# One step more of lag in a software-pipelined attention: transposes, products with v and cluster ranking

## The chip, the core and the metric

The kernel runs on one core of one Trainium2 chip. The time is device microseconds (us) for one execution. The kernel before takes 794.31 us (median of 3 runs, 794.3 to 795.95). TensorE is called PE here, VectorE DVE, ScalarE ACT, GpSimd POOL, and SP is the engine that issues most DMAs.

## The reference, cut to what matters

```python
# q, k, v: (2, 8, 768, 64); centroids: (8, 16, 64)
q_assign = argmax(q_n . c_n)            # the cluster of each query, out of 16
k_assign = argmax(k_n . c_n)
scores = where(q_assign == k_assign, q k^T / 8, -1e9)
attn = softmax(scores)
x = (attn v)  ->  (1536 tokens, 512)
h = x @ w_in;  g = P(h) / Q(h);  x = g @ w_out            # first MLP, 2048 hidden
y = (silu(x @ w_gate) * (x @ w_val)) @ w_out2             # second MLP, 1536 hidden
```

All matmuls are made exact to float32 by splitting each operand into a high and a low part, so that most products are three or four matmuls.

## The kernel before

There are 16 heads (2 batches of 8). Each head has T = 6 query tiles of 128 rows against all 768 keys, so the attention is a sequence of NT = 96 tiles. One loop over `step` (lines 583, 803, 1011 and 1210) is written out once for each engine, and each engine runs its instructions strictly in that written order; semaphores join the engines. Step s handles different stages of different tiles:

- PE, from line 1210: the scores of tile s (four matmuls, L1226 and L1229; they wait for the exponentials of tile s-2), then six transposes of the probabilities of tile s-LAG (L1239), then a third of a product with v (L1254, L1256), then in some steps the cluster work of a later head.
- DVE: the row maximum of tile s (`neg_max`, L1035), once in three steps the sum and the reciprocal of three row sums (L1046, L1049, at step s divisible by three), then the low half of the transposed tile s-LAG in two instructions (`probT_lo`, L1057), and once in three steps the sum of the two parts of a finished product with v (`x_raw`, L1066).
- ACT: the exponentials of tile s-1 (L811), the high half of the transposed tile s-LAG in two instructions (`probT_hi`, L829), and once in three steps a copy of half the product with v (`x_part`, L839).
- POOL: at steps divisible by three it scales three probability tiles by their reciprocals (L589); at steps divisible by six it splits q and k of a later head (L597 to L606); at step 3 of six it splits v (L614, L617); some steps split weights of the first MLP (L624, L626); and once in twelve steps it splits the finished x of a pair of heads (L636, L638; the "x pair").

A half head is three tiles. `pv_at(step)` gives the half head g and the third whose product with v runs in a step: it starts PV_LAG = LAG + 3 steps after the half head's first scores. The first half of the transposes of a tile waits until DVE has read the first half of the tile before it out of the same PSUM bank (line 1238, semaphore s_pT_lo), and its second half likewise. The first third of a product waits for `x_raw` of the product before it (line 1251).

The cluster ranking of a head h is a chain of stages, placed by `head_at(step, stage)`: the stage runs at step 6h + late + stage - 18. Stage 6 and the step after it are the products with the cluster centres (L1313, PE), stage 8 sums them and takes the maximum (L1072 and L1074, DVE), 9 marks the maximum (L1080, DVE), 10 transposes the marks (L1278, PE), 11 ranks them (L819 on ACT, L1292 on PE) and 12 makes the cluster rows (L1024 and L1026, DVE, at the front of the step), which SP then copies to where the scores of head h read them (L390). For heads 3 and up, before the change, the centre products run at steps 0 and 1 of six, the sum at step 2, the marks at 3, their transposes at 4, the ranking at 5 and the rows at 0.

`prob` has six buffers. The exponentials of tile i overwrite the buffer of tile i-6 and wait for its transposes (line 809). They are issued in step i+1 of ACT.

At steps 96 to 103 PE also runs the first hidden units of the first MLP in pieces of six matmuls of 512 columns (TAIL_CHUNKS, L1109 to L1111). The loop ends three steps after the last product with v. The first result of the MLP (`first_result(0)`, line 1140) waits for all `x_raw` sums, since it writes the PSUM bank of the products with v. After that PE runs two long phases of matmuls.

Of the kernel before, what the change touches and what calls it, by code (L numbers as in the profile page):

```python
# [21 lines left out]
def build_program(nc, q, k, v, centroids, w_in, w_out1, a, b, w_gate, w_val, w_out2, out):  # L22
# [9 lines left out]
    HALF = T // 2  # L32
    HC = HALF * P
    NG = NH * 2
# [110 lines left out]
    def loaded(h):  # L145

        return qk_raw_3 if h == 3 else qk_raw[h % 3]
# [106 lines left out]

    R_LAG = 3
    COPIES, CLROWS = 16 * 6, 16 * T
    LAG = 5
    PV_LAG = LAG + HALF
    V_STEP = 3
    X_STEP, LAST_X_STEP = 5, 2  # L260
    PREP_LEAD = 18
    FIRST_STEP = -PREP_LEAD
    S_SPLIT, S_CEN, S_LOGIT, S_SUM, S_TOP, S_TOPT, S_RANK, S_CLUSTER = 0, 2, 6, 8, 9, 10, 11, 12
# [4 lines left out]
    def head_at(step, stage):  # L268


        for h in range(NH):
            late = -4 * (h == 1) + (h == 2 and stage <= S_SUM)
            if T * h + late == step + PREP_LEAD - stage:
                return h
        return None

    def tile_at(step):
        return step if 0 <= step < NT else None

    def pv_at(step):  # L280

        g, third = (step - PV_LAG) // HALF, (step - PV_LAG) % HALF
        return (g, third) if 0 <= g < NG else (None, None)

    def copied(h):
        return s_copy[h % 3], COPIES * (h // 3 + 1)
# [23 lines left out]
    def x_pair(x, h):  # L310
        col = (h // H) * S
        return x[:, (h % H) // 2, col:col + S]
# [51 lines left out]
    with block:  # L364
# [114 lines left out]
        def _(pool):  # L479
# [20 lines left out]
            def did(ins, signal):  # L500
                last["count", signal] = last.get(("count", signal), 0) + 1
                last["signal"] = signal
                ins.then_inc(signal, 1)

            def finish_last():


                pool.wait_ge(last["signal"], last["count", last["signal"]])

            def mlp1(n):  # L510


                i = n % 2
                if n < N1:
                    pool.wait_ge(s_lin, n + 1)
                    did(g.tensor_tensor(den[i][:, :], den[i][:, :], mag[i][:, :], ALU.mult), s_quad)  # L516
                for u, when in w1_split_at.items():
                    if when == n:
                        pool.wait_ge(s_w1_in[u], 32)
                        did(g.tensor_scalar(w1_hi[u][:, :], w1_raw[u][:, :], 1.0, 1.0, ALU.mult, ALU.mult),  # L520
                            s_w1hi)
                        pool.wait_ge(s_w1hi, u - POOL_UNITS + 1)
                        did(g.tensor_tensor(w1_lo[u][:, :], w1_raw[u][:, :], w1_hi[u][:, :].bitcast(F32),
                                            ALU.subtract), s_w1lo)
                for b, when in enumerate(T_SUM_AT):
                    if when == n:
                        token_sums(0, b)
                for m, when in enumerate(W_SUM_AT):
                    if when == n:
                        weight_sums(m)  # L530
                for k, when in enumerate(T_LO_AT):
                    if when == n:
                        token_lo(0, k)
                for m, when in enumerate(W_LO_AT):
                    if when == n:
                        weight_lo(m)
# [46 lines left out]
            for step in STEPS:  # L583
                if (step - HALF) % HALF == 0 and 0 <= (step - HALF) // HALF < NG:
                    half = (step - HALF) // HALF
                    pool.wait_ge(s_inv, half + 1)
                    for n in range(HALF):
                        i = (half * HALF + n) % T
                        did(g.tensor_scalar(prob[i][:, :], prob[i][:, :], row_inv[:, i:i + 1], 1.0,  # L589
                                        ALU.mult, ALU.mult), s_norm)  # L590
                h = head_at(step, S_SPLIT)
                if h is not None and h >= 2:
                    i = h % 3
                    if h == 2:
                        pool.wait_ge(s_qklo, 2)
                    pool.wait_ge(s_qk_in[i], 32 * (h // 3 + 1))
                    did(g.tensor_scalar(loaded(h)[0:D, :], loaded(h)[0:D, :], QSCALE, 1.0,  # L597
                                        ALU.mult, ALU.mult), s_qscale)
                    pool.wait_ge(s_qscale, h - 1)
                    if h == 3:  # L600
                        pool.wait_ge(*copied(0))
                        pool.wait_ge(s_logit, 1)
                    did(g.tensor_scalar(qk_hi[i][:, :], loaded(h)[:, :], 1.0, 1.0, ALU.mult, ALU.mult),
                        s_qkhi)
                    pool.wait_ge(s_qkhi, h + 1)
                    did(g.tensor_tensor(qk_lo[i][:, :], loaded(h)[:, :], qk_hi[i][:, :].bitcast(F32),  # L606
                                        ALU.subtract), s_qklo)

                h = (step - V_STEP) // T
                if (step - V_STEP) % T == 0 and 0 <= h < NH:  # L610
                    pool.wait_ge(s_v_in[h % 2], 16 * (h // 2 + 1))
                    if h >= 2:
                        pool.wait_ge(s_pv, 2 * (h - 1))
                    did(g.tensor_scalar(v_split[h % 2][:, :, 0, :], v_raw[h % 2][:, :, :], 1.0, 1.0,  # L614
                                    ALU.mult, ALU.mult), s_vhi)
                    pool.wait_ge(s_vhi, h + 1)
                    did(g.tensor_tensor(v_split[h % 2][:, :, 1, :], v_raw[h % 2][:, :, :],  # L617
                                    v_split[h % 2][:, :, 0, :].bitcast(F32), ALU.subtract), s_vlo)

                for u, when in pool_split_at.items():  # L620
                    if when != step:
                        continue
                    pool.wait_ge(s_w1_in[u], 32)
                    did(g.tensor_scalar(w1_hi[u][:, :], w1_raw[u][:, :], 1.0, 1.0, ALU.mult, ALU.mult), s_w1p_hi)  # L624
                    pool.wait_ge(s_w1p_hi, u + 1)
                    did(g.tensor_tensor(w1_lo[u][:, :], w1_raw[u][:, :], w1_hi[u][:, :].bitcast(F32),  # L626
                                    ALU.subtract), s_w1p)
                g1, third = pv_at(step - X_STEP)
                if pv_at(step - LAST_X_STEP) == (NG - 1, HALF - 1):
                    g1, third = NG - 1, HALF - 1  # L630
                if third == HALF - 1 and g1 % 4 == 3:
                    pool.wait_ge(s_xsum, g1 + 1)
                    finish_last()
                    h = g1 // 2
                    xh, xl, raw = x_pair(x_hi, h), x_pair(x_lo, h), x_pair(x_raw, h)
                    did(g.tensor_scalar(xh, raw, 1.0, 1.0, ALU.mult, ALU.mult), s_xhi)  # L636
                    pool.wait_ge(s_xhi, h // 2 + 1)
                    did(g.tensor_tensor(xl, raw, xh.bitcast(F32), ALU.subtract), s_xlo)  # L638
                    finish_last()

                if step in TAIL:
                    mlp1(TAIL[step])
# [15 lines left out]
        def _(sc):  # L658
# [144 lines left out]
            for step in STEPS:  # L803

                i = tile_at(step - 1)
                if i is not None:
                    sc.wait_ge(s_max, i + 1)
                    if i >= T:
# [3 lines left out]
                                 ps[:, bank:bank + 2, 0:HC], ACT.Exp, bias=neg_max[:, i % T:i % T + 1],  # L812
                                 accum_out=row_sum[:, i % T, 0:1]).then_inc(s_exp, 1)
                h = head_at(step, S_RANK)
                if h is not None:
                    sc.wait_ge(s_topT, h + 1)
                    if h == 0:
# [3 lines left out]
                                 ACT.Copy).then_inc(s_topT_in, 1)  # L821
                i = tile_at(step - LAG)
                if i is not None:
# [50 lines left out]
        def _(ve):  # L874
# [136 lines left out]
            for step in STEPS:  # L1011
# [25 lines left out]
                if (step - HALF) % HALF == 0 and 0 <= (step - HALF) // HALF < NG:  # L1037
# [11 lines left out]
                    v_.reciprocal(row_inv[:, c:c + HALF], row_den[:, c:c + HALF]).then_inc(s_inv, 1)  # L1049
                i = tile_at(step - LAG)  # L1050
                if i is not None:
# [47 lines left out]
        def _(pe):  # L1099
# [110 lines left out]
            for step in STEPS:  # L1210
                i = tile_at(step)
                if i is not None:
# [18 lines left out]
                    last.then_inc(s_score, 1)  # L1231
                i = tile_at(step - LAG)
                if i is not None:
# [143 lines left out]
```

## Time and profile before

| | |
|---|---|
| median of the runs | 794.31 us |
| the profiled execution | 794.28 us, of it a span of 792.5 us |
| PE busy | 781.2 us (99%) |
| DVE busy | 571.9 us (72%) |
| ACT busy | 517.3 us (65%) |
| POOL busy | 522.7 us (66%) |
| attention | about 16 to 264 us of the span |
| first and second MLP | about 264 us to the end |

A timeline row has the start and the busy time in us, then engine, line, operation, output and inputs, and the count of like instructions merged. A bracket at its end says how long the engine sat idle before it and what ended that. A row of matmuls counts each up to its modelled end, so the starts are what to compare: the time from one start to the next is the time that the work takes on the engine.

### The profile page before, as it was taken

The numbers are of one execution on the slowest core, as the hardware profiler recorded it, in microseconds if no ns is written. First come the engines' busy times: TensorE is split into PE (matmuls) and PEld (weight loads), VectorE is DVE, ScalarE is ACT, GpSimd is POOL, SyncE is SP. The second block draws the span as 40 slices with busy tenths as digits, with TensorE's granted clock in tenths as the row PEclk, the third lists the DMA queues.
The fourth block names the chain that finished last, engine by engine and source line by source line (L and its number), as shares of the span: only waits on it lengthen the run. The fifth ranks groups of instructions, "written<-read, shape, count | busy, mean of one in ns | idle before, by whom it ended". The sixth has DMA issues, their size and how long they took to land.

```text
span 792.5 us, 12617 instructions
## 1 busy us (share of the span) xinstructions
PE 781.2 (99%) x4204; PEld 697.7 (88%) x4204; DVE 571.9 (72%) x1043; ACT 517.3 (65%) x957; POOL 522.7 (66%) x457
## 2 busy tenths in 40 slices
PE   8999999999999999999999999999999999999998
PEld 7799999999998888888888888899999999999997
DVE  5899999999997888778777777745445545554453
ACT  4888888888887787777767889744444444333322
POOL 4767988998575799322222288888889876655620
PEclk8999999999999999999999999999999999999999
DMA  8776555454310700000000011241111114111102
GB/s 206 180 199 162 143 140 125 116 145 121 85 60 19 221 28 0 1 1 1 1 1 0 1 55 54 66 147 50 32 54 53 37 45 134 54 28 53 28 1 80
DMA packets 57681, 57.92 MB, mean 73 GB/s; under 512 B 6608, under 2 KB 44304, under 8 KB 57616
## 3 DMA queue, kind: packets, MB, share of 16 engines
q1 hardware_dynamic: 57376, 56.52, 26.6%
q8 instruction: 34, 0.56, 0.3%
q10 hardware_dynamic: 240, 0.59, 0.3%
q14 instruction: 31, 0.25, 0.1%
HBM read 33.59 MB, written 3.15 MB: 46 GB/s over the span
## 4 chain that ended last, share of the span: by engine, by line
PE 87%; DVE 8%; issue 2%; ACT 2%; DMA 0%; DVEq 0%; ACTq 0%
PE ps L1111 18%; PE ps L1109 18%; PE ps L1110 18%; PE ps L1239 6%; PE ps L1204 4%; PE ps L1205 4%; PE ps L1203 4%; DVE neg_max L1035 3%; DVE probT_lo L1057 3%; PE ps L1254 3%; PE ps L1226 3%; PE ps L1256 3%; PE ps L1313 2%; PE ps L1229 2%; ACT prob L811 1%
## 5 line engine op out<-in xcount | busy, mean ns | idle before, releaser
L516 POOL TENSOR_TENSOR den<-den,mag 128x512 f32<-128x512 f32 x48 | 62.3, 1298 | 121.8 <-ACT den L689 121.6
L1111 PE MATMUL ps<-x_hi,w_lo 128*128 128x512 f32 (+1 forms) x384 | 139.5, 363 | 0.0
L1109 PE MATMUL ps<-x_hi,w_hi 128*128 128x512 f32 (+1 forms) x384 | 139.4, 363 | 0.0
L1110 PE MATMUL ps<-x_lo,w_hi 128*128 128x512 f32 (+1 forms) x384 | 139.3, 363 | 0.0
L575 POOL TENSOR_TENSOR w_lo<-w_raw,w_hi 128x768 fp32r<-128x768 f32 (+1 forms) x48 | 101.6, 2125 | 56.4 <-ACT w_hi L742 56.4
L589 POOL TENSOR_SCALAR prob<-prob,row_inv 128x768 f32<-128x768 f32 x96 | 85.6, 907 | 39.2 <-DVE row_inv L1049 38.7
L829 ACT ACTIVATE probT_hi<-ps 128x384 fp32r<-128x384 f32 x192 | 84.2, 489 | 25.9 <-PE ps L1239 24.2
L1057 DVE TENSOR_TENSOR probT_lo<-ps,probT_hi 128x384 fp32r<-128x384 f32 x192 | 96.8, 545 | 5.3 <-ACT probT_hi L829 4.0
L1035 DVE TENSOR_REDUCE neg_max<-ps 128x1 f32<-128x768 f32 x96 | 91.1, 950 | 8.8 <-PE ps L1229 8.5
L811 ACT ACTIVATE prob<-ps,neg_max 128x768 f32<-128x768 f32 x96 | 86.8, 905 | 10.8 <-DVE neg_max L1035 10.1
L1239 PE MATMUL ps<-ident,prob 128*128 128x128 f32 x576 | 81.7, 277 | 4.4 <-DVE probT_lo L1057 4.1
L1239 PEld LDWEIGHTS ps<-ident,prob 128*128 128x128 f32 x576 | 65.6, 140 | 17.0 <-issue 9.9
L1109 PEld LDWEIGHTS ps<-x_hi,w_hi 128*128 128x128 f32 x384 | 72.1, 188 | 8.2
L1110 PEld LDWEIGHTS ps<-x_lo,w_hi 128*128 128x128 f32 x384 | 72.1, 188 | 8.2
L1111 PEld LDWEIGHTS ps<-x_hi,w_lo 128*128 128x128 f32 x384 | 72.1, 188 | 7.5
L1111 PE MATMUL ps<-g_hi,w_lo 128*128 128x512 f32 x192 | 74.8, 390 | 0.0
L1110 PE MATMUL ps<-g_lo,w_hi 128*128 128x512 f32 x192 | 74.8, 390 | 0.0
L1109 PE MATMUL ps<-g_hi,w_hi 128*128 128x512 f32 x192 | 74.8, 390 | 0.0
L1254 PE MATMUL ps<-probT_hi,v_split 128*128 128x384 f32 x192 | 72.5, 378 | 0.0
L763 ACT ACTIVATE act_hi<-ps 128x384 fp32r<-128x384 f32 x48 | 23.6, 492 | 64.6 <-DVE ps L992 43.7
L1256 PE MATMUL ps<-probT_lo,v_split 128*128 128x384 f32 x192 | 64.6, 337 | 0.0
L959 DVE TENSOR_TENSOR sum<-ps,gate 128x384 f32<-128x384 f32 x24 | 13.4, 557 | 68.9 <-PE ps L1111 68.9
(145 smaller groups left out, 1987.5 us busy)
## 6 DMA issues: line engine op xcount, KB each, us to landing
k_hihi<-qk_hi SPq DMA_DIRECT2D x32, 192.0 KB, 4.0
w_raw<-in_moe_w_gate SPq DMA_DIRECT2D x48, 128.0 KB, 2.3
w_raw<-in_moe_w_val SPq DMA_DIRECT2D x48, 128.0 KB, 2.5
w_raw<-in_moe_w_in SPq DMA_DIRECT2D x16, 256.0 KB, 3.7
w_raw<-in_moe_w_out SPq DMA_DIRECT2D x16, 256.0 KB, 5.0
qk_raw<-in_q SPq DMA_DIRECT2D x16, 192.0 KB, 3.4
q_hilo<-qk_hi SPq DMA_DIRECT2D x16, 192.0 KB, 3.4
qk_low<-qk_hi SPq DMA_DIRECT2D x16, 192.0 KB, 4.5
```

Of the source, the lines that this page charges most:

```text
L575: did(g.tensor_tensor(lo[:, wave, :], raw[:, wave, :], hi[:, wave, :].bitcast(F32), ALU.subtract), s_w2lo)
L589: did(g.tensor_scalar(prob[i][:, :], prob[i][:, :], row_inv[:, i:i + 1], 1.0, ALU.mult, ALU.mult), s_norm)
L811: s.activation(prob[i % T][:, :].rearrange("p (c n) -> p c n", c=2), ps[:, bank:bank + 2, 0:HC], ACT.Exp, bias=neg_max[:, i % T:i % T + 1] ...
L829: s.activation(probT_hi[g % 2][:, n * HALF:(n + 1) * HALF, c:c + P], ps[:, PT_BANK + n, 0:HC].rearrange("p (k n) -> p k n", k=HALF), ACT.C ...
L1035: v_.tensor_reduce(neg_max[:, i % T:i % T + 1], ps[:, bank:bank + 2, 0:HC], AX.XY, ALU.max, negate=True).then_inc(s_max, 1)
L1057: v_.tensor_tensor(probT_lo[g % 2][:, keys, c:c + P], ps[:, PT_BANK + n, 0:HC].rearrange("p (k n) -> p k n", k=HALF), probT_hi[g % 2][:, k ...
L1109: mm(dst, hi, m_hi, start=start, stop=False)
L1110: mm(dst, hi, m_lo, start=False, stop=False)
L1111: return mm(dst, lo, m_hi, start=False, stop=stop)
L1239: last = transpose(ps[:, PT_BANK + n, kt % HALF * P:(kt % HALF + 1) * P], prob[i % T][:, kt * P:(kt + 1) * P], ident[:, :])
L1254: mm(ps[:, O_BANK, 0:HC], vv, probT_hi[g % 2][:, kt, :], start=(kt == 0), stop=False)
L1256: last = mm(ps[:, O_BANK, 0:HC], vv, probT_lo[g % 2][:, kt, :], start=False, stop=(kt == T - 1))
```

## The change

Four things: LAG becomes 6, so that transposes, the halves of the transposed tile and the products with v come one step later (PV_LAG follows). The x pair of POOL comes one step after the end of its product with v instead of five, which puts it at step 9 of twelve, where v is split, in place of step 0 of twelve, where q and k are split. The special case of the last pair falls away; it stays at step 105. And for heads 2 and up all stages from the centre products on come one step later; for head 2 those up to the sum were so already.

```diff
-    LAG = 5
+    LAG = 6
     PV_LAG = LAG + HALF
     V_STEP = 3
-    X_STEP, LAST_X_STEP = 5, 2
+    X_STEP = 1
...
         for h in range(NH):
-            late = -4 * (h == 1) + (h == 2 and stage <= S_SUM)
+            late = -4 * (h == 1)
+            if h >= 2:
+                late = 1 if stage >= S_LOGIT else int(h == 2)
             if T * h + late == step + PREP_LEAD - stage:
                 return h
...
                 g1, third = pv_at(step - X_STEP)
-                if pv_at(step - LAST_X_STEP) == (NG - 1, HALF - 1):
-                    g1, third = NG - 1, HALF - 1
                 if third == HALF - 1 and g1 % 4 == 3:
```

## Rows read from the trace of the kernel before

**Rows 1.** Who waited for whom, 40 to 219 us: us in total, times, longest.

```profile
PE ps L1239 <- DVE probT_lo L1057: 3.5, 12, 0.4
```

**Rows 2.** Timeline of PE, the transposes of steps 43 to 49: start us, us.

```profile
116.57 0.82 PE L1239 MATMUL ps<-ident,prob 128*128 128x128 f32 x6
119.31 0.82 PE L1239 MATMUL ps<-ident,prob 128*128 128x128 f32 x6
121.37 0.82 PE L1239 MATMUL ps<-ident,prob 128*128 128x128 f32 x6
123.92 0.92 PE L1239 MATMUL ps<-ident,prob 128*128 128x128 f32 x6 [0.34 <-DVE probT_lo L1057]
126.31 0.82 PE L1239 MATMUL ps<-ident,prob 128*128 128x128 f32 x6
128.48 0.90 PE L1239 MATMUL ps<-ident,prob 128*128 128x128 f32 x6
131.31 0.82 PE L1239 MATMUL ps<-ident,prob 128*128 128x128 f32 x6
```

**Rows 3.** Timeline of DVE, steps 40 to 47.

```profile
110.42 1.01 DVE L1057 TENSOR_TENSOR probT_lo<-ps,probT_hi 128x384 fp32r<-128x384 f32 x2
...
112.05 0.96 DVE L1035 TENSOR_REDUCE neg_max<-ps 128x1 f32<-128x768 f32 x1
...
119.51 0.96 DVE L1035 TENSOR_REDUCE neg_max<-ps 128x1 f32<-128x768 f32 x1 [0.26 <-PE ps L1229]
120.50 1.02 DVE L1057 TENSOR_TENSOR probT_lo<-ps,probT_hi 128x384 fp32r<-128x384 f32 x2
121.44 0.36 DVE L1072 TENSOR_TENSOR ps<-ps,logit_lo 128x192 f32<-128x192 f32 x1
...
122.10 0.95 DVE L1035 TENSOR_REDUCE neg_max<-ps 128x1 f32<-128x768 f32 x1
122.97 0.15 DVE L1046 TENSOR_REDUCE row_den<-row_sum 128x3 f32<-128x6 f32 x1
...
123.24 0.99 DVE L1057 TENSOR_TENSOR probT_lo<-ps,probT_hi 128x384 fp32r<-128x384 f32 x2
124.15 0.35 DVE L1080 TENSOR_TENSOR is_top<-ps,top 128x192 f32<-128x192 f32 x1
124.42 0.95 DVE L1035 TENSOR_REDUCE neg_max<-ps 128x1 f32<-128x768 f32 x1
125.28 1.01 DVE L1057 TENSOR_TENSOR probT_lo<-ps,probT_hi 128x384 fp32r<-128x384 f32 x2
...
126.67 0.94 DVE L1035 TENSOR_REDUCE neg_max<-ps 128x1 f32<-128x768 f32 x1
```

**Rows 4.** Timeline of the end of attention, PE and DVE, steps 102 to 103 and after.

```profile
261.98 0.39 PE L1109 MATMUL ps<-x_hi,w_hi 128*128 128x512 f32 x1
...
263.41 0.47 PE L1109 MATMUL ps<-g_hi,w_hi 128*128 128x512 f32 x1
...
262.70 0.56 DVE L1066 TENSOR_TENSOR x_raw<-ps,x_part 64x384 f32<-64x384 f32 x1 [1.59 <-ACT x_part L839]
```

**Rows 5.** Timeline of PE at the start, step 4.

```profile
20.69 0.62 PE L1226 MATMUL ps<-k_hihi,q_hilo 128*128 128x384 f32 x2 [0.21 <-ACT prob L811]
...
22.84 0.42 PE L1278 MATMUL ps<-ident,is_top 128*96 128x128 f32 x2 [1.17 <-DVE is_top L1080]
```

**Rows 6.** Timeline of PE, transposes of steps 86 and 92, where no cluster work is left.

```profile
221.45 0.82 PE L1239 MATMUL ps<-ident,prob 128*128 128x128 f32 x6
...
234.35 0.82 PE L1239 MATMUL ps<-ident,prob 128*128 128x128 f32 x6
```

**Rows 7.** Timelines of POOL, PE and SP: scaling behind an x pair, and cluster rows sent.

```profile
139.53 2.69 POOL L589 TENSOR_SCALAR prob<-prob,row_inv 128x768 f32<-128x768 f32 x3
...
140.91 0.82 PE L1239 MATMUL ps<-ident,prob 128*128 128x128 f32 x6
...
118.84 4.62 SPq L390 DMA_DIRECT2D qk_low<-clusterT  x6
```

## The prediction

> **What bounds the kernel now.** I read the page first: PE is busy for nearly the whole span, also in attention. Then I asked the waits of the attention for PE's rows alone. What stands there is small and of one kind: the transposes waiting for the low half of the tile before, in the same PSUM bank [rows 1]. No wait for POOL's scaled probabilities and none for a DMA. So PE is the bound engine, and each gap is DVE running just behind it. The timeline of one head then shows where. From one start of the transposes to the next, a plain step takes PE 2.06 us (119.31 to 121.37), a step with half of the centre products 2.74 (116.57 to 119.31), the step with the mark transposes 2.39 (123.92 to 126.31), the ranking step 2.17 (126.31 to 128.48). Step 3 of six, 121.37 to 123.92, takes 2.55 for work of 2.06: a wait of 0.49 us in each head. A whole head takes 14.74 us (116.57 to 131.31) [rows 2].
>
> DVE's costs, start to start [rows 3]: row maximum 0.87 (122.10 to 122.97), sum and reciprocal 0.27 (122.97 to 123.24), the two low halves 0.94 (120.50 to 121.44) or 0.91 behind the reciprocal (123.24 to 124.15), centre sum and maximum 0.66 (121.44 to 122.10), marks 0.27 (124.15 to 124.42). The two low halves with the `x_raw` that lies between them and the next maximum take 1.39 (125.28 to 126.67), but 1.63 in another head (110.42 to 112.05). Two lags join the engines: the maximum starts 0.20 after the transposes of its step (119.31, 119.51), and the next transposes start 0.68 after the low halves (123.24, 123.92) [rows 2, 3].
>
> **The change part by part.** No instruction is added or removed. What counts is where PE stands idle, at the end, at the start, in the 13 heads that run with cluster work beside them, and in the last 12 tiles, which run without.
>
> *The end.* All PE work is the same, so an idle PE is the whole cost. Before, behind the last third of the last product with v, PE still has a piece of the MLP from 261.98 on, and under it ACT and DVE make the last `x_raw` (262.70). The first MLP result starts at 263.41, 1.43 us later, at nearly no wait [rows 4]. After the change the product ends one step later, at step 104, and there is no piece at 104: it has run ahead of it. So the 1.43 us is bare, less a few hundredths that were bare before: +1.4 us. Nothing later gives it back, since PE has no gap in the MLP that follows. The last x pair stays at step 105 of POOL and waits for the same `x_raw`; the MLP chain moves with it.
>
> *The start.* PE waits 1.17 us for the marks of head 2 in step 4 [rows 5]. They are now transposed in step 5, behind the scores of that step, so this wait mostly goes. Next late is the chain of scores, maximum and exponentials, on which the scores two tiles on wait (it shows as the 0.21 in the same group), and the first transposes have left this stretch, so there is less to fill it with. Bounds 0 and -1.17; I take -0.4, nearer to none, for that second reason.
>
> *Thirteen heads.* Scores, sum and reciprocal stay at their steps; transposes, low halves, `x_raw` and all cluster stages move by one. So the new thing is the order on DVE: `x_raw` now stands right ahead of the steps with the reciprocal, and the centre sum right behind one. Working it through, with time 0 at the transposes of step 2 of six: a centre step gives transposes 3 at 2.74 and maximum 3 at 2.94; low halves 3 at 2.94 + 0.87 + 0.27 = 4.08; transposes 4 at 2.74 + 2.06 = 4.80 (DVE would allow 4.76). Maximum 4 at 4.08 + 0.91 + 0.66 = 5.65, low halves 4 at 6.52, so transposes 5 at 6.52 + 0.68 = 7.20 where PE was ready at 6.86: a wait of 0.34. Maximum 5 at 6.52 + 0.94 + 0.27 = 7.73, low halves 5 at 8.60, maximum 0 at 8.60 + 1.39 = 9.99 or + 1.63 = 10.23, low halves 0 at 11.13 or 11.37. Transposes 0 at 7.20 + 2.39 = 9.59; transposes 1 at the later of 9.59 + 2.17 = 11.76 and 11.81 or 12.05; and the next step 2 at + 2.83 (the 128.48 to 131.31 of rows 2) = 14.64 or 14.88. The mean is 14.76. The same working on the order of before gives: low halves 2 at 1.07, sum 2.01, maximum 3 at 2.67, low halves 3 at 3.81, transposes 4 at 4.49, then 6.88, 9.05, 11.88 and 14.62, where the trace has 14.74. So it is short by 0.12 there, and I compare working with working: +0.14 a head, 13 x 0.14 = +1.8 us. Ends: against the row itself only +0.02 (+0.3 us in all); and the long `x_raw` in every head +0.26 (+3.4 us).
>
> A rule of the Trainium skill bears on the two values of `x_raw` (VectorE: DVE Perf Modes, section "Two Vector instructions with no wait between them"): a Vector instruction whose operands begin in another group of 32 partitions than those before it is held until all earlier ones have finished, otherwise it may start sooner. By that rule the 0.24 us belongs to every second head, the one whose x lies in partitions 64 to 127, which the mean above takes; the two heads of the rows agree. If every change of instruction were held, the time with the end of each would be some 0.08 us more at each of four boundaries ahead of transposes 5, and 13 heads would cost about 4 us more; the row of 122.10, busy for 0.95 and followed after 0.87, speaks against it.
>
> *Last 12 tiles.* Before, two half heads take 12.90 us (221.45 to 234.35) [rows 6], 6.45 each against PE's 3 x 2.06 = 6.18. Working: before, `x_raw` and the reciprocal lie in different steps, waits 0 or 0.13; after, low halves to low halves over both is 1.39 or 1.63 plus 0.87 + 0.27, which puts the transposes at 4.28 or 4.52 against PE's 4.12, waits 0.16 or 0.40. The difference of the means is 0.21, over 4 half heads 0.8; as the row shows that DVE already costs 0.27 each, I take +0.5, between 0 and 0.8.
>
> *What costs nothing.* Prob's buffers: with a lag of 6 the exponentials of a tile overwrite the tile whose transposes ran in the PE step before, and ACT has read those before it comes to them in its own order. POOL: before, scaling behind an x pair begins at 139.53 and its first tile is done some 0.9 later, just ahead of its transposes at 140.91 [rows 7]; PE does not wait for it, so taking the pair out of that step gains nothing, and the new place has a step more of slack. Were that cover gone, the cost would be up to a scaled tile, 0.9 us a pair. Cluster rows: DVE makes them ahead of the centre products that lie before 116.57, so one step later is before 119.31, and SP sends them from 118.84 [rows 2, 7]; the DMAs may start 0.5 later and are read first at step 48, 128.48. Behind them on SP stand loads a head ahead. The centre products wait for the rows in the same step on both sides. The first MLP's weights that wait for the last transposes move by one step, well ahead of use.
>
> The sum: 1.4 - 0.4 + 1.8 + 0.5 = +3.3 us. The profiled execution took 794.28 (span 792.5), practically the median of 794.31, so 797.6 us.
>
> **The rivals.** *Steady part neutral.* The waits only change places, as the working leaves open (its error on before is nearly its result). Then end and start remain: +1.0, 795.3 us. For it: DVE's total is the same. Against: the `x_raw` directly ahead of the reciprocal.
>
> *Faster.* The centre sum no longer stands ahead of the reciprocal, which is what makes the wait of 0.49. If the moved sum is hidden wholly behind the two centre steps of PE, this wait goes in 13 heads: -6.4, and with end and start -5.4, 788.9 us. It decides from 0.08 us saved a head on (1.0 / 13). For it: step 3's DVE work falls. Against: step 4 then has the sum and PE has no extra work in steps 3 and 4, where it used to have the mark transposes in 4.
>
> *The change does less than it says.* Head 2's centre stages and the last x pair stand where they were; that leaves the rest as worked out and has no time of its own.
>
> *More than worked out.* The waits of both new places, transposes 5 and 1, come in full in every head with the long `x_raw`: 13 x 0.26 and 0.8, 799.6 us or a little more.
>
> **How the numbers follow.** Forecast 0.58, neutral 0.22, faster 0.12, more than worked out 0.08. 0.2%, 1.6 us, is about what a measurement of this kernel can tell from no change. Slower by over that: the forecast nearly whole, the last case and a little of the neutral one, 0.64. Within: most of the neutral, with edges of the forecast and the faster one, 0.26. Faster 0.10. The range goes from 794.2, the low edge of the neutral case, to 800.0, the sum of the upper ends (1.4 + 3.4 + 0.8 = 5.6 and no gain at the start, 799.9); the faster case is left out.
>
> **What would show it.** In the profile after: the first MLP result starting about 1.4 us after the last product with v, with PE idle; no 1.17 us ahead of the mark transposes of head 2; in each head a wait of 0.3 to 0.5 at step 5 of six in place of the one at step 4, a second one ahead of step 1 in every second head, and a head at 14.8 to 14.9 us. If a head takes 14.6 or less, or PE waits for scaled probabilities, the prediction is wrong at that step.

## The result and the profile after

The changed kernel takes 803.63 us (median of 4 runs, 802.64 to 803.81) where the kernel before, run beside it, takes 795.13 (794.3 to 795.96): a ratio of 1.0102, interval 1.0082 to 1.0122. It is slower, as forecast, but by 8.5 us instead of 3.3, and outside the range (794.2 to 800.0). Executions of one kernel fall into groups some 1.8 us apart (here two of before at 794.3 and two at 795.95), so a median of few executions can move by that much. The profiled execution has a span of 800.9 against 792.5; all stretches below are read from one profiled execution of each kernel.

Five starts on PE divide the attention: the first scores, the scores of steps 12, 84 and 95, and the first MLP result. They are counted here so that the first row maximum stands at 16.57 in each trace.

| | first scores | step 12 | step 84 | step 95 | first MLP result |
|---|---|---|---|---|---|
| before | 15.62 | 39.20 | 216.18 | 240.22 | 263.40 |
| after | 15.66 | 38.81 | 218.00 | 242.73 | 271.69 |

After the first MLP result nothing differs: it comes 8.29 later, and the last matmul of L1109 stands at 788.73 against 780.39, 8.34 later. So the whole loss lies in the attention. With a lag one step longer, PE has one tile's transposes and one third of a product less behind it whenever it comes to given scores. That is 1.36 us of work, which must be added to the start and taken from the end before idle time is compared. It comes from a tile where PE does not wait: transposes at 260.25, product at 260.83, next work at 261.61, all three in the fence below.

| stretch | forecast | measured |
|---|---|---|
| start, to the scores of step 12 | -0.4 | -0.39 + 1.36 = +0.97 |
| steps 12 to 84 (12 of the 13 heads) | +1.8 in 13 | 179.19 - 176.98 = +2.21 |
| steps 84 to 95 | +0.5 | 24.73 - 24.04 = +0.69 |
| end, from the scores of step 95 | +1.4 | 28.96 - 23.18 - 1.36 = +4.42 |
| sum | +3.3 | +8.29 |

One product of the ranking (L1292, 0.11 us) goes with the ranking's shift: in after it stands behind the scores of step 12 instead of ahead of them, and likewise at step 84. So some +1.08 of the start and +0.58 of steps 84 to 95 is time lost; the sum stays.

The end is where the larger part went. PE of after, timeline (start, busy, engine, line; the bracket is idle time and what ended it), the rows that answer to [rows 4]:

```profile
257.41 0.92 PE L1239 MATMUL ps<-ident,prob 128*128 128x128 f32 x6 [0.63 <-DVE probT_lo L1057]
...
260.25 0.82 PE L1239 MATMUL ps<-ident,prob 128*128 128x128 f32 x6
260.83 0.42 PE L1254 MATMUL ps<-probT_hi,v_split 128*128 128x384 f32 x1
...
261.61 0.39 PE L1109 MATMUL ps<-x_hi,w_hi 128*128 128x512 f32 x1
...
265.31 0.41 PE L1254 MATMUL ps<-probT_hi,v_split 128*128 128x384 f32 x1 [2.15 <-DVE x_raw L1066]
...
271.68 0.47 PE L1109 MATMUL ps<-g_hi,w_hi 128*128 128x512 f32 x1 [1.26 <-DVE x_raw L1066]
```

Only the last of these three waits was in the forecast. (In the same stretch before has one listed wait, 0.47 us at 243.05.) Why the middle one is there, DVE's timeline of after says:

```profile
259.42 0.68 DVE L925 SCALAR_TENSOR_TENSOR den<-den,ps 128x512 f32<-128x512 f32 x1
260.14 0.69 DVE L929 SCALAR_TENSOR_TENSOR ps<-den,ps 128x512 f32<-128x512 f32 x1
260.87 0.76 DVE L933 SCALAR_TENSOR_TENSOR ps<-num,par,ps 128x512 f32<-128x512 f32 x1
261.53 0.68 DVE L944 TENSOR_TENSOR num<-num,ps 128x512 f32<-128x512 f32 x1
262.25 0.75 DVE L946 SCALAR_TENSOR_TENSOR num<-num,par,ps 128x512 f32<-128x512 f32 x1
262.95 0.69 DVE L953 TENSOR_TENSOR g_lo<-ps,g_hi 128x512 fp32r<-128x512 f32 x1
263.56 1.01 DVE L1057 TENSOR_TENSOR probT_lo<-ps,probT_hi 128x384 fp32r<-128x384 f32 x2
264.60 0.56 DVE L1066 TENSOR_TENSOR x_raw<-ps,x_part 64x384 f32<-64x384 f32 x1
```

And before, where `x_raw` of the last product but one stood in step 100, ahead of the same work:

```profile
255.23 1.02 DVE L1057 TENSOR_TENSOR probT_lo<-ps,probT_hi 128x384 fp32r<-128x384 f32 x2 [0.76 <-ACT probT_hi L829]
256.33 0.56 DVE L1066 TENSOR_TENSOR x_raw<-ps,x_part 64x384 f32<-64x384 f32 x1
256.92 0.69 DVE L925 SCALAR_TENSOR_TENSOR den<-den,ps 128x512 f32<-128x512 f32 x1
```

The six instructions of the first MLP are put into the loop at fixed steps, counted from NT (`TAIL = {NT + 2: 0, NT + 4: 1}`, and TAIL_LOG likewise). They did not move with the lag. The last low halves and `x_raw` moved to step 101, behind the block of step 100: 4.14 us of DVE (259.42 to 263.56) that nobody waits for yet stand ahead of the two instructions that PE's last product waits for. The first wait, 0.63, is of the same kind: the low halves before it begin at 256.71, behind two MLP instructions of step 98.

The start. PE of after in steps 4 to 6 and at step 12, answering to [rows 5], and SP's issue of DMAs:

```profile
20.66 0.62 PE L1226 MATMUL ps<-k_hihi,q_hilo 128*128 128x384 f32 x2 [0.20 <-ACT prob L811]
...
22.53 0.62 PE L1226 MATMUL ps<-k_hihi,q_hilo 128*128 128x384 f32 x2 [0.19 <-ACT prob L811]
...
24.41 0.59 PE L1226 MATMUL ps<-k_hihi,q_hilo 128*128 128x384 f32 x2 [0.42 <-ACT prob L811]
...
38.80 0.59 PE L1226 MATMUL ps<-k_hihi,q_hilo 128*128 128x384 f32 x2 [0.93 <-issue]
```

```profile
32.10 1.41 SPq L387 DMA_DIRECT2D qk_low<-qk_lo  x1
33.55 3.89 SPq L392 DMA_DIRECT2D qk_low<-clusterT  x6
```

DVE of after, which makes these rows, and the same copies and scores before:

```profile
27.64 0.28 DVE L1026 TENSOR_SCALAR clusterT<-ps 96x128 fp32r<-96x128 f32 x1
```

```profile
33.69 3.98 SPq L390 DMA_DIRECT2D qk_low<-clusterT  x6
...
39.20 0.52 PE L1226 MATMUL ps<-k_hihi,q_hilo 128*128 128x384 f32 x2
```

The 1.17 of [rows 5] is gone, and the wait moved to the scores that wait for exponentials, as forecast. But a new 0.93 stands ahead of the scores of step 12, the first that read head 2's cluster rows. The rows are ready on DVE at 27.92; their six copies are issued from 33.55 to 37.44, because SP is behind with its own work. They are issued no later than before (33.69 to 37.67). What changed is PE: with 1.47 us less work behind it (1.36 and the 0.11 of the ranking product) it could begin these scores 1.32 us earlier than before (38.81 - 0.93 against 39.20), and their rows are not there yet.

Nor had PE gained anything by then. The scores of step 10 start at 34.26 before and at 32.92 in after: -1.34 + 1.36 = +0.02, where the forecast had -0.4.

A head in the steady part, PE's transposes of after, answering to [rows 2]:

```profile
119.78 0.82 PE L1239 MATMUL ps<-ident,prob 128*128 128x128 f32 x6
122.52 0.82 PE L1239 MATMUL ps<-ident,prob 128*128 128x128 f32 x6
124.67 0.92 PE L1239 MATMUL ps<-ident,prob 128*128 128x128 f32 x6
127.12 0.92 PE L1239 MATMUL ps<-ident,prob 128*128 128x128 f32 x6
129.50 0.82 PE L1239 MATMUL ps<-ident,prob 128*128 128x128 f32 x6
131.70 0.91 PE L1239 MATMUL ps<-ident,prob 128*128 128x128 f32 x6
134.53 0.82 PE L1239 MATMUL ps<-ident,prob 128*128 128x128 f32 x6
...
144.12 0.82 PE L1239 MATMUL ps<-ident,prob 128*128 128x128 f32 x6
146.70 0.92 PE L1239 MATMUL ps<-ident,prob 128*128 128x128 f32 x6
149.54 0.71 PE L1239 MATMUL ps<-ident,prob 128*128 128x128 f32 x5
```

From step 2 of six, in one head: 2.74, 4.89, 7.34, 9.72, 11.92, 14.75; the next head takes 15.01 (134.53 to 149.54), with 2.58 between steps 0 and 1 (144.12 to 146.70) where the first has 2.20. The mean is 14.88 against the 14.74 of [rows 2].

### The profile page after: what moved, and what is told of

Its sections match the earlier page's. It is cut to its first block, busy times and chain, and to the rows that moved or that the text cites. A ratio compares the mean times of both kernels' runs of the same rounds, so it can differ in the third digit from the quotient of the medians.

```text
span 800.9 us, 12617 instructions
## 1 busy us (share of the span) xinstructions
PE 785.7 (98%) x4204; PEld 696.9 (87%) x4204; DVE 571.6 (71%) x1043; ACT 517.9 (65%) x957; POOL 523.4 (65%) x457
## 4 chain that ended last, share of the span: by engine, by line
PE 88%; DVE 7%; issue 3%; ACT 1%; DMA 0%; DVEq 0%
PE ps L1109 18%; PE ps L1111 18%; PE ps L1110 18%; PE ps L1239 6%; PE ps L1204 4%; PE ps L1205 4%; PE ps L1203 4%; PE ps L1226 3%; DVE probT_lo L1057 3%; PE ps L1254 3%; PE ps L1229 3%; PE ps L1256 3%; PE ps L1313 3%; DVE neg_max L1035 2%; PE ps L1278 0%
## 5 line engine op out<-in xcount | busy, mean ns | idle before, releaser
L1109 PE MATMUL ps<-x_hi,w_hi 128*128 128x512 f32 (+1 forms) x384 | 139.2, 362 | 0.0
L1109 PEld LDWEIGHTS ps<-x_hi,w_hi 128*128 128x128 f32 x384 | 72.1, 188 | 8.3
L1109 PE MATMUL ps<-g_hi,w_hi 128*128 128x512 f32 x192 | 74.8, 389 | 1.3 <-DVE x_raw L1066 1.3
```

Source lines behind the costliest of these rows:

```text
L1109: mm(dst, hi, m_hi, start=start, stop=False)
```

## The experiments

Theory A throughout: the loss is the place of a few DVE instructions in DVE's order, at the end and in each head, and SP's queue at the start. All kernels compute the whole reference. The first four were run beside 8 runs of before (median 795.9), the next four beside 21 (794.26), the last four beside 22 (794.28); against 794.3 the ratios of the first four would be up to 0.2% higher.

**The MLP's steps one later.** The changed kernel with

```diff
-    TAIL = {NT + 2: 0, NT + 4: 1}
-    TAIL_LOG = {NT + 3: 0, NT + 5: 1}
+    TAIL = {NT + 3: 0, NT + 5: 1}
+    TAIL_LOG = {NT + 4: 0, NT + 6: 1}
```

> The changed kernel with the first MLP's vector work inside the attention loop (TAIL, TAIL_LOG) one step later; PE's pieces stay where they are. Theory A (DVE's queue order: since the change, six MLP instructions of step 100 stand ahead of the low halves and x_raw of step 101): x_raw of half head 30 comes some 4 us sooner, the 2.15 us of PE ahead of the first third of the last product goes, and the wait of about 0.8 us ahead of the transposes of step 100; 1.3 us at the first MLP result stays. About 3 us less than the changed kernel, some 800.6 us. Theory B (the lag itself costs it, because one tile more is open at the end): PE still waits for x_raw at that place, no more than 1 us less, 802.6 to 803.6 us.

Measured 799.35, ratio 1.0050 (1.0032 to 1.0067), span 797.5. It is 4.3 us under after's median, more than the 3 expected. The waits of 2.15 and 0.63 are gone, and DVE has the old order again, before's with one step more:

```profile
260.13 1.02 DVE L1057 TENSOR_TENSOR probT_lo<-ps,probT_hi 128x384 fp32r<-128x384 f32 x2 [0.76 <-ACT probT_hi L829]
261.23 0.56 DVE L1066 TENSOR_TENSOR x_raw<-ps,x_part 64x384 f32<-64x384 f32 x1
261.83 0.69 DVE L925 SCALAR_TENSOR_TENSOR den<-den,ps 128x512 f32<-128x512 f32 x1
```

From step 95 to the first MLP result it takes 25.91: 25.91 - 23.18 - 1.36 = +1.37, which is 3.05 less than in after. It is the forecast's +1.4 for the end, and the 1.26 ahead of the first MLP result is still there. So the forecast for the end was right for a kernel in which the MLP's steps had moved, which this was not.

**The pieces ahead of the MLP one later as well.** The same, and

```diff
-    TAIL_CHUNKS = {NT + n: ((2 * n) // DC, (2 * n) % DC) for n in range(AHEAD * DC // 2)}
+    TAIL_CHUNKS = {NT + 1 + n: ((2 * n) // DC, (2 * n) % DC) for n in range(AHEAD * DC // 2)}
```

> The changed kernel with TAIL, TAIL_LOG and also PE's MLP pieces one step later, so that the end has the alignment of the kernel before. Theory A: all three waits of the end go (0.8, 2.15 and 1.3 us), about 4.2 us less than the changed kernel, some 799.4 us, and the first MLP result starts within 23.5 us of the last tile's scores (23.2 before, 29.0 changed) plus the 1.4 us of one tile's transposes and thirds. Theory B: the first MLP result gains the 1.3 us alone, 802.3 us.

Measured 798.56, 1.0043 (1.0026 to 1.0060), span 796.5: step 95 to the result 25.24, so +0.70 is left of the end. With a piece of work at step 104 the last `x_raw` is covered again; what the 0.70 is was not followed up.

**Sum and reciprocal one step later.** The changed kernel with the row sums, reciprocals and the scaling on POOL at steps 1 and 4 of six:

```diff
-                if (step - HALF) % HALF == 0 and 0 <= (step - HALF) // HALF < NG:
-                    half = (step - HALF) // HALF
+                if (step - HALF - 1) % HALF == 0 and 0 <= (step - HALF - 1) // HALF < NG:
+                    half = (step - HALF - 1) // HALF
```

> The changed kernel with the row sums, reciprocals (DVE) and the scaling (POOL) one step later, so that x_raw is no longer right ahead of the step with the reciprocal. Theory A (order on DVE): a head goes from 14.89 back to 14.7 us, the last 12 tiles from 24.7 to about 24.1 us, together about 2.7 us less than the changed kernel, 800.9 us. Rival (POOL is what PE waits for at step 5 of six, as the profile's releaser says): scaling starts a step later, the wait grows by up to 2 us a head, and the kernel is over 10 us slower than the changed one.

Measured 807.29, 1.0147 (1.0131 to 1.0162), slower than theory A's 800.9 by 6.4 us. Steps 12 to 84 did shorten by 1.23 and 84 to 95 by 0.46, in the direction of theory A. But step 12 comes 6.3 later, which neither theory had:

```profile
31.34 0.82 POOL L599 TENSOR_SCALAR qk_raw<-qk_raw 64x768 f32<-64x768 f32 x1 [5.63 <-DMA qk_raw<-in_k]
...
34.95 2.67 POOL L591 TENSOR_SCALAR prob<-prob,row_inv 128x768 f32<-128x768 f32 x3
```

The scaling of step 7 now stands behind the split of q and k of step 6, which waits for its load, and PE waits 5.36 us for it. The edit moved a step past a blocked instruction on POOL; it was the wrong test of the steady part, and the tenth run replaces it.

**SP's queue at the start.** The changed kernel with two small loads out of the way of head 2's cluster rows:

```diff
-            sp.dma_start(a_raw, a[None, :].to_broadcast([P, 4])).then_inc(s_par_in, 16)
-            sp.dma_start(b_raw, b[None, :].to_broadcast([P, 2])).then_inc(s_par_in, 16)
...
                 send_cluster(h - 1)
+                if h == 3:
+                    sp.dma_start(a_raw, a[None, :].to_broadcast([P, 4])).then_inc(s_par_in, 16)
+                    sp.dma_start(b_raw, b[None, :].to_broadcast([P, 2])).then_inc(s_par_in, 16)
```

> The changed kernel with SP's two small loads of a and b moved from ahead of the third load of v to behind the six cluster row DMAs of head 2. Theory A (SP's issues, back to back from 14 to 41 us, set when the cluster rows of head 2 land, and so the scores of step 12): these DMAs are issued about 1 us sooner and the 0.93 us of PE ahead of the scores of step 12 goes, 0.9 us less than the changed kernel in the trace at that place. Rival (the rows wait for the cluster work, which the change puts a step later): no change of that wait.

Measured 802.87, 1.0089 (1.0074 to 1.0104), 0.8 below after's median. The wait of 0.93 is gone:

```profile
37.42 0.59 PE L1227 MATMUL ps<-k_hihi,q_hilo 128*128 128x384 f32 x2
```

The scores of step 12 come 1.10 earlier than in after (37.71 on the common count), which leaves -0.13 of the start's +0.97. How much this wait is worth differs from one execution to the next: three other kernels here have the start of after unchanged (the first, second and tenth run), and their profiled executions wait 0.56, 0.14 and 1.05 us at this place. The span of the profiled execution, 801.0, shows no gain. What took it is a fall of the clock at the end, told below under the hardware: step 95 to the result takes 30.52 here, 28.96 in after.

**The ranking's shift alone.** The kernel before with

```diff
-            late = -4 * (h == 1) + (h == 2 and stage <= S_SUM)
+            late = -4 * (h == 1)
+            if h >= 2:
+                late = 1 if stage >= S_LOGIT else int(h == 2)
```

> The kernel before with one part of the change alone: the cluster ranking of heads 2 and up one step later (stages from the centre products on), lag of the transposes 5 as before. Theory A (the steady cost is an order on DVE: what counts is which DVE work stands next to which): with the ranking shifted and the low halves not, the centre sum stands behind the x_raw and the mark transposes fall into the ranking step; working it through as in the prediction gives a head some 0.3 us longer than before's (about 15.0 where before has 14.7), so steps 12 to 84 about 3 to 4 us longer, the rest unchanged: about 798.5. Rival B (the two shifts cost separately, each for itself, and the ranking's is the small one): within 0.5 us of before, 795.5.

Measured 796.95, 1.0039 (1.0024 to 1.0055). Steps 12 to 84 take 179.31, +2.33; step 12 comes at 38.80, 0.40 earlier than before's, 0.11 of it the ranking product that now comes later; the rest is unchanged. The loss per head is 0.19, less than the 0.3 worked out, and the time lies between theory A's 798.5 and rival B's 795.5; at 2.7 us over before it is well outside B's 0.5. With a lag of 5 the later ranking does gain at the start, some 0.3 of the forecast's 0.4.

**The lag alone.** The kernel before with

```diff
-    LAG = 5
+    LAG = 6
...
-    X_STEP, LAST_X_STEP = 5, 2
+    X_STEP = 1
```

> The kernel before with the other part alone: transposes and products with v one step later (LAG 6, the x pair one step behind its product), the ranking where it was. Theory A: the centre sum, the reciprocal and the x_raw now stand in neighbouring steps of DVE, all ahead of low halves that PE waits for; worked through, a head takes about 15.4 us, 0.65 more than before's 14.7; 12 heads give +8, the end +5.8 as in after, the last tiles +0.7: first MLP result some 14 us later than before's, about 808 to 810. The shift of the ranking then takes back more than half of what the later transposes cost. Rival B (costs add up separately): after's own time, about 803.6, less at most 0.5.

Measured 807.67, 1.0171 (1.0158 to 1.0185); steps 12 to 84 take 183.37, +6.39, or 0.53 a head, where 0.65 was worked out; the time is just under theory A's 808 to 810 and rules out rival B's 803.6. DVE shows what the shift of the ranking spares:

```profile
123.24 1.01 DVE L1055 TENSOR_TENSOR probT_lo<-ps,probT_hi 128x384 fp32r<-128x384 f32 x2
124.28 0.56 DVE L1064 TENSOR_TENSOR x_raw<-ps,x_part 64x384 f32<-64x384 f32 x1
124.88 0.37 DVE L1070 TENSOR_TENSOR ps<-ps,logit_lo 128x192 f32<-128x192 f32 x1
...
125.55 0.95 DVE L1033 TENSOR_REDUCE neg_max<-ps 128x1 f32<-128x768 f32 x1
126.41 0.15 DVE L1044 TENSOR_REDUCE row_den<-row_sum 128x3 f32<-128x6 f32 x1
126.60 0.18 DVE L1047 RECIPROCAL row_inv<-row_den 128x3 f32<-128x3 f32 x1
126.69 0.99 DVE L1055 TENSOR_TENSOR probT_lo<-ps,probT_hi 128x384 fp32r<-128x384 f32 x2
```

From one pair of low halves to the next 3.45 us, with `x_raw`, the centre sum and the reciprocal all between them, and PE waits 0.75 for it in this head. So the two parts do not add: +2.33 and +6.39 alone, +2.21 together. In DVE's order the ranking's shift belongs to the later lag; it is no cost of its own there.

The start has the same pattern. The lag alone costs it 1.57 (39.41 - 39.20 + 1.36) without any wait for SP, and of this +1.42 is there at step 10 already (34.32 - 34.26 + 1.36): the work that the lag takes away ahead of these scores does not bring them forward. No listed wait accounts for it (PE waits 1.15 us for the marks of head 2 here, 1.17 before), so its cause stays open. In the whole change the later ranking takes that loss back, to the +0.02 above.

**POOL's x pairs alone.** The kernel before with `X_STEP = 2` for all pairs and no case for the last.

> The kernel before with GpSimd's x pairs alone moved (X_STEP 2 in place of 5 for all, no special case of the last): the pair of each two heads is made three steps earlier on POOL, on a step without scaling. Theory A (the move of the x pair has no part in the loss): within 0.5 us of before, 795. Rival (the pair sat where it hurt, or now holds up the scaled probabilities or the v split): a wait of PE for prob, or of the product with v, of 0.5 to 1 us in each of 8 pairs, 4 to 8 us slower.

Profiled execution: span 792.7 against 792.5, steps 12 to 84 177.31 against 176.98, and no new wait for `prob` or for a product. (The scores of step 12 wait 0.64 us, though the start is that of before: in this execution the first row maximum came at 15.59 instead of 16.57, and SP's row copies no earlier, up to 37.65. So SP has next to no slack there before the change either.) The median is 796.20 (1.0015, 1.0006 to 1.0024). Its ten runs fall into five at 794.43 to 794.55 and five at 796.19 to 796.56; of the 21 of before beside it 16 are at 793.77 to 794.59 and five at 795.86 or more. The interval thus comes from how often the upper group came, and the lower one is 0.4 above before's. I take from it that the x pairs cost under 0.5 us and not the 4 to 8 of the rival; whether they change how often the upper group comes is not settled.

**Reciprocal behind the low halves, on before.** The kernel of the run before, and on DVE the block of row sum and reciprocal moved below the two low halves of its step:

```diff
-                if (step - HALF) % HALF == 0 and 0 <= (step - HALF) // HALF < NG:
-                    ...
                 i = tile_at(step - LAG)
                 if i is not None:
                     ...
+                if (step - HALF) % HALF == 0 and 0 <= (step - HALF) // HALF < NG:
+                    ...
```

> The kernel before, x pairs as in the run before this (X_STEP 2), and on DVE the row sum and its reciprocal put behind the two low halves of the same step, where they stood ahead of them. Theory A (0.27 us of row sum and reciprocal ahead of the low halves is what makes the wait of 0.49 us at step 3 of six): that wait mostly goes from the 14 heads, while POOL gets the reciprocals 0.9 us later and its scaled tiles can be late instead; worked through, head 14.65 to 14.75 where before has 14.75, and the first MLP result 0.9 us earlier: 794.2, between 793 and 795.5. Rival B (the low halves wait for ACT's high halves anyway, so order on DVE does not matter): 795.1, no difference. Rival C (scaled tiles come late): PE waits for prob at the first transposes of a half head, 0.2 us in each of 30, 5 to 6 us slower.

Measured 793.52, 0.9992 (0.9982 to 1.0003). Steps 12 to 95 take 200.30 against 201.02, so 0.72 less, in line with theory A; steps 12 to 84 alone 176.65 against 176.98. The listed waits of 3.5 us of [rows 1] are all gone, and yet that stretch is only 0.33 shorter. The time is 0.7 lower in the median, which the interval cannot tell from no change. POOL's scaled tiles are not late.

**Everything mended.** The changed kernel with the edits of the first, second and fourth run, and the reciprocal behind the low halves.

> The changed kernel with everything that the runs so far name as its cost mended: the first MLP results' steps one later and the pieces of the MLP that run ahead one later, the loads of a and b behind head 2's cluster rows on SP, and row sum and reciprocal behind the two low halves on DVE. Theory A (the loss is the sum of the order on DVE at the end, the order on DVE in the steady part, and SP's queue at the start, and nothing else): the end gives back 4.4 us (as in the second run), the start about 1.0 (as in the fourth), the steady part and last tiles about 2.5 (from 0.18 to about 0 a head): 803.6 - 7.9 = 795.7, that is, at before's time within 1 us, with PE's waits at the end under 1.5 us. Rival B (a later lag costs by itself, since the pipeline drains one step later): 798.0 or more.

Measured 795.29, 1.0006 (0.9996 to 1.0017): theory A's 795.7, not rival B's 798. The first MLP result comes at 264.52, 1.12 behind before's: end 25.24 - 23.18 - 1.36 = 0.70, steps 12 to 84 0.23, 84 to 95 0.26, start 37.77 - 39.20 + 1.36 = -0.07.

This kernel has an edit that helps before too, though, the reciprocal behind the low halves. Against the run before this one, which has it with a lag of 5, the median is 1.8 us more (795.29 and 793.52), and the stretches are longer by 0.56 (177.21 and 176.65), 0.65 (24.30 and 23.65) and 0.70 at the end. So of the lag's cost most is mended, but some 1.8 us remain that no experiment here explains; that the lag costs something by itself is not excluded.

**Reciprocal behind the low halves, on after.** The changed kernel with this one edit.

> The changed kernel with one edit: row sum and reciprocal behind the two low halves of the same step on DVE. Theory A (the waits of the changed kernel at steps 5 and 1 of six come from the 0.27 us of row sum and reciprocal, ahead of low halves that PE waits for): head 14.67 where after has 14.89, so steps 12 to 84 about 2.2 us shorter (177.0), 84 to 95 at 24.0, end and start as in after: 800.9 to 801.5. Rival B (the x_raw ahead of the reciprocal, not the reciprocal, makes the wait): 803.6, no difference, head 14.89.

Measured 800.78, 1.0071 (1.0050 to 1.0092). Steps 12 to 84 take 177.03 against after's 179.19 and before's 176.98, steps 84 to 95 24.28. In the changed kernel the place of 0.3 us of DVE work (123.70 to 123.99 in after), ahead of low halves or behind them, is worth 2.16 of the 2.21 us lost in steps 12 to 84. On the kernel before the same edit was worth 0.33, so it is the later lag that makes this place dear. In steps 84 to 95 it is worth as much on both (0.45 and 0.39), so the loss there has another cause, which stays open. The waits view of this kernel and of after over 39 to 219 us (us in total, times, longest) holds a warning:

```profile
PE ps L1239 <- DVE probT_lo L1044: 3.4, 12, 0.3
PE ps L1226 <- issue: 1.0, 1, 1.0
```

```profile
PE ps L1226 <- issue: 0.9, 1, 0.9
PE ps L1313 <- DVE clusterT L1026: 0.5, 1, 0.5
```

The faster one shows 3.4 us of waits, like the 3.5 of [rows 1]; the slower one shows none for the low halves. Its waits, spread over several steps, are too short to be listed. Start to start finds them.

**Head 2 alone, and a version meant to beat both.** The kernel before with only head 2's ranking later at all stages, and the loads of a and b as in the fourth run; the eleventh run has the eighth run's edits as well.

```diff
-            late = -4 * (h == 1) + (h == 2 and stage <= S_SUM)
+            late = -4 * (h == 1) + (h == 2)
```

> A version meant to beat both: the kernel before, with row sum and reciprocal behind the low halves (as in the eighth run, 0.7 us), and of the ranking's shift only head 2's, for which PE waits 1.17 us in step 4, with the loads of a and b behind head 2's cluster rows so that SP does not hold the scores of step 12. Theory A: the start gives back 0.4 us by its working (the scores then wait for the exponentials), up to 1.17: 793.1 to 792.4 where the eighth run had 793.5. Rival B: the start's wait only moves, 793.5.

> The kernel before with the start's part of the change alone, without what held it up: only head 2's ranking one step later, and the loads of a and b behind head 2's cluster rows on SP. Theory A (the later ranking of head 2 is a gain at the start that SP's queue cut short in the changed kernel): scores of step 12 at 38.8 or earlier after the first maximum at 16.57, where before has 39.20, PE's wait for the marks gone: 793.9, between 793.3 and 794.1. Rival B (the wait moves to the scores that wait for the exponentials): no difference, 794.3.

Measured 797.73 (1.0033, 1.0021 to 1.0044) and 798.20 (1.0039, 1.0023 to 1.0055). Both theories fall. PE of the twelfth run:

```profile
28.03 0.38 PE L1293 MATMUL ps<-topT,rank 128*128 128x256 f32 x1
30.10 0.27 PE L1314 MATMUL ps<-cenT,qk_hi 128*128 128x64 f32 x1 [1.69 <-DVE clusterT L1027]
...
31.90 1.48 PE L1240 MATMUL ps<-ident,prob 128*128 128x128 f32 x6
```

Head 3's centre products, at step 6, write where head 2's ranking is read, and wait until DVE has made head 2's cluster rows, which now happens in step 7. So head 2 cannot be moved alone; the change moves the heads behind it too, and has no such wait. The scores of step 12 come 3.7 us later than before (42.94 against 39.20), more than the wait of 1.69: behind it the granted clock is 0.89 from 28 to 32 us, 0.50 to 36 and 0.76 to 40, where before has 1.00.

## Why the prediction was wrong

*The end, +1.4 forecast, +4.4 measured.* The step that failed is "the MLP chain moves with it". It does not: its steps are counted from NT, and I had not followed DVE's written order through steps 100 and 101. The wait that I did work out is there (1.26 us bare, +1.37 as a whole in the first run); the missing 3.0 is DVE's block of step 100 ahead of the last low halves and `x_raw`. The first run shows it: moving one pair of constants shortens this stretch by 3.05 us.

*The start, -0.4 forecast, +0.97 measured.* Two steps failed. The gain of PE is not there: the wait for the marks went, but by step 10 the change has +0.02, not -0.4. That is the upper of the two bounds that the prediction gave (0 and -1.17), and it had named a reason, that the first transposes have left the stretch; alone the later ranking gains (-0.40, with a lag of 5), and alone the lag loses 1.42 at this place. The other step is the one that costs the cluster rows at nothing: I looked at DVE's rows and SP's issues in a later head [rows 7], and said that the rows are read well after. For head 2 SP's queue is full from the first load on. Its copies are not later than before, but PE comes 1.32 us earlier and waits 0.93 us for them. In the fourth run this wait is gone (-0.13 left).

*The heads, +0.14 forecast, +0.18 measured* (2.21 / 12). By its own steps: transposes 4 at 4.80 and measured 4.89, 5 at 7.20 and 7.34, 0 at 9.59 and 9.72, 1 at 11.81 and 11.92 with the short `x_raw`, and 2 at 14.64 and 14.75. Every second head is longer by 0.26 (15.01), as the two rows of `x_raw` had it (0.24). This trace agrees with the rule of the Trainium skill that the prediction names (VectorE: DVE Perf Modes, section "Two Vector instructions with no wait between them"): the longer heads are those whose x lies in partitions 64 to 127. One head, from 20 to 26, takes 15.51, with a wait of 0.54 us for cluster rows at 73.56, which before does not have there; without it the loss is (2.21 - 0.54) / 12 = 0.14 a head. A wait took the place of another, as forecast, and the tenth run shows that it hangs on the reciprocal. The rival that the centre sum's going would win 6.4 us is wrong for the reason given: step 3 now takes 2.15 (122.52 to 124.67), near its 2.06, but step 4, which got the sum, takes 2.45.

*The last tiles, +0.5 forecast, +0.69 measured*, within its 0 to 0.8. The size is right; the mechanism is not confirmed, since the reciprocal behind the low halves leaves +0.63 (24.28 with a lag of 6, 23.65 with 5). *The x pairs at nothing*: right to 0.5 us by the seventh run. *Prob's buffers at nothing*: right, no such wait is in the trace.

The range failed for the same reason as the forecast: its upper end added the upper ends of the costs that I had, and the largest cost, the MLP's block at the end, was not among them.

## What to carry to other kernels

When a lag in a software pipeline changes, list every piece of work whose step is a constant, and for each in-order engine write out the new order around it: what did not move is now ahead of what did. A step at the start or the end of the loop needs its own look at each queue, the one that issues DMAs too, since the steady part says nothing about its slack there. And weigh an instruction by what is queued behind it: 0.3 us of row sum and reciprocal ahead of the work that PE waits for cost 2.2 us over 12 heads in the changed kernel, and 0.3 us in the kernel before.

## What the runs showed of the hardware

PE's clock fell behind waits of 1.2 to 2.2 us, in some executions and not in others. In the fourth run, behind the wait of 2.15 us at the end, matmuls of 512 columns go from 0.39 to 0.63 us:

```profile
263.95 0.41 PE L1255 MATMUL ps<-probT_hi,v_split 128*128 128x384 f32 x1 [2.15 <-DVE x_raw L1067]
...
264.86 0.63 PE L1110 MATMUL ps<-x_hi,w_hi 128*128 128x512 f32 x1
```

The granted clock is 0.82 in 262 to 266 us and 0.76 in 266 to 270, so a part of it at 1.2 GHz, where after, with the same 2.15 us of idle time, has 1.00 throughout. The stretch is 1.56 us longer for it, more than the 1.10 that the edit had won. The third run has the same (0.62 from 270 to 274). In the eighth run's profiled execution it fell at the start: 0.65 from 24 to 28 us behind the wait for the marks, where before has 1.00 with a like wait, and this execution took 795.00 where most of that kernel took 793.2 to 793.8. Before's own runs lie at about 794.2 or about 796. A fall of the clock is not shown as the cause: of the upper group some have a mean granted clock of 0.994 (795.9 us), but others 1.000 (796.2 to 796.4), where the lower group has 0.996 to 0.998; no trace of such a run was taken. A wait of PE can thus cost more than it shows, or not: 2.15 us cost 1.56 more in the fourth run and nothing more in after, and with 1.69 us in the twelfth run step 12 came 3.7 us later.
